# Attention and two dense layers: the product of the last 64 keys in two column halves, and q's rounding and remainder sooner where short units begin

## The reference

```python
scores = scale * np.matmul(q, k.transpose(0, 1, 3, 2))
...
scores = scores + bias.transpose(2, 0, 1)[None, :, :, :]
scores = scores - np.max(scores, axis=-1, keepdims=True)
attn = np.exp(scores)
attn = attn / (np.sum(attn, axis=-1, keepdims=True) + 1e-09)
x = np.matmul(attn, v)            # then the heads side by side: 2304 x 512
h = x @ w_in;  x = (h - np.tanh(h)) @ w_out             # 512 -> 2048 -> 512
g = x @ w_gate
out = (g * (1.0 / (1.0 + np.exp(-g))) * (x @ w_val)) @ w_out2   # 512 -> 1536 -> 512
```

## Time and profile before

| | us |
|---|---|
| median of 3 runs | 1214.85 |
| lowest, highest | 1213.22, 1215.16 |
| the profiled execution | 1216.6 |
| its span, first to last instruction | 1214.7 |
| PE busy | 1179.5 |
| DVE busy | 613.9 |
| ACT busy | 569.4 |
| POOL busy | 527.7 |

### The profile page before, as it was taken

One profiled execution on the slowest core, in us unless ns is written; L12 is line 12 of the kernel. 1 busy time (PEld: TensorE's weight loads), 2 busy tenths in 40 slices (PEclk: granted clock), 3 DMA queues, 4 the chain that ended last, 5 costly groups with the idle time before them and its releaser, 6 DMA issues.

```text
span 1214.7 us, 20186 instructions
## 1 busy us (share of the span) xinstructions
PE 1179.5 (97%) x7320; PEld 1080.2 (89%) x7320; DVE 613.9 (51%) x1377; ACT 569.4 (47%) x1163; POOL 527.7 (43%) x584
## 2 busy tenths in 40 slices
PE   6789999999999999999999999999999999999998
PEld 2356799999999998999999999999999999999998
DVE  8967888766666666666666444321212212121111
ACT  7977676665565556555655544321212112121212
POOL 1057577756565657778777522111111111111111
PEclk9999999999999999999999999999999999999999
DMA  6889565353444335545555433100000000000000
GB/s 199 259 255 266 162 183 152 109 140 109 128 131 125 108 89 159 133 134 138 153 137 139 138 131 130 53 27 27 27 1 27 26 26 26 1 26 1 26 1 26
DMA packets 77763, 125.46 MB, mean 103 GB/s; under 512 B 17120, under 2 KB 40672, under 8 KB 77664
## 3 DMA queue, kind: packets, MB, share of 16 engines
q1 hardware_dynamic: 77664, 124.16, 35.1%
HBM read 104.07 MB, written 20.05 MB: 102 GB/s over the span
## 4 chain that ended last, share of the span: by engine, by line
PE 89%; DVE 5%; ACT 2%; POOL 2%; issue 2%; DMA 0%; DVEq 0%; POOLq 0%; ACTq 0%
PE ps_y L1556 16%; PE ps_h L1537 15%; PE ps_s L1672 12%; PE ps_y L1683 12%; PE ps_s L1454 6%; PE ps_h L1672 6%; PE ps_pt L1672 6%; PE ps_pt L1508 5%; PE ps_pt L1473 5%; DVE feat L1139 3%; PE ps_pt L1537 1%; PE ps_pt L1483 1%; ACT feat L807 1%; PE ps_y L1495 1%; DVE prob L1174 1%
## 5 line engine op out<-in xcount | busy, mean ns | idle before, releaser
L772 POOL TENSOR_TENSOR fr<-tanh_b,fr 128x384 fp32r<-128x384 f32 x72 | 73.2, 1016 | 377.9 <-ACT fr L1066 377.9
L1556 PE MATMUL ps_y<-fr,wbuf 128*128 128x384 f32 x1152 | 230.0, 337 | 0.0
L1537 PE MATMUL ps_h<-fr,wbuf 128*128 128x384 f32 x1056 | 206.3, 338 | 0.3 <-DVE fr L1224 0.3
L1556 PEld LDWEIGHTS ps_y<-fr,wbuf 128*128 128x128 f32 x1152 | 198.2, 188 | 0.7 <-POOL fr L709 0.7
L1537 PEld LDWEIGHTS ps_h<-fr,wbuf 128*128 128x128 f32 x1056 | 181.7, 188 | 1.3 <-issue 0.8
L837 ACT ACTIVATE prob<-prob,negmax 128x576 f32<-128x576 f32 (+1 forms) x160 | 124.0, 775 | 122.9 <-DVE negmax L1174 122.2
L704 POOL TENSOR_SCALAR prob<-prob,rowinv 128x576 f32<-128x576 f32 (+1 forms) x160 | 134.0, 839 | 89.1 <-DVE rowinv L1185 88.9
L1683 PE MATMUL ps_y<-wbuf,fr 128*128 128x512 f32 x648 | 161.1, 393 | 0.0
L709 POOL TENSOR_TENSOR fr<-g_b,fr 128x384 fp32r<-128x384 f32 x96 | 100.6, 1047 | 139.2 <-ACT fr L868 139.2
L1683 PEld LDWEIGHTS ps_y<-wbuf,fr 128*128 128x128 f32 x648 | 120.5, 188 | 22.1 <-POOL fr L772 0.2
L1190 DVE TENSOR_TENSOR wbuf<-ps_pt,wbuf 128x512 fp32r<-128x512 f32 (+1 forms) x136 | 91.6, 673 | 52.4 <-ACT wbuf L851 48.0
(11 more groups left out here) (134 smaller groups left out, 1948.7 us busy)
## 6 DMA issues: line engine op xcount, KB each, us to landing
biasb<-bias_scratch SPq DMA_DIRECT2D x64, 288.0 KB, 3.2
raw<-k_t SPq DMA_DIRECT2D x59, 288.0 KB, 3.0
biasb<-bias_scratch SPq DMA_DIRECT2D x64, 216.0 KB, 2.9
bias_scratch<-w_raw SPq DMA_DIRECT2D x72, 144.0 KB, 3.4
biasb<-bias_scratch SPq DMA_DIRECT2D x64, 144.0 KB, 3.0
w_raw<-w_chunks SPq DMA_DIRECT2D x16, 512.0 KB, 5.1
prob<-w_chunks SPq DMA_DIRECT2D x8, 768.0 KB, 4.3
raw<-v_p SPq DMA_DIRECT2D x36, 160.0 KB, 2.3
```

What stands on the lines that cost most here:

```text
L1537: mm = eng.matmul(hidden_bank(u, c)[:, 0:TOK], w[:, cols], x[:, d, :], start=d == 0 and i == 0, stop=d == KC - 1 and i == 2)
L1556: mm = eng.matmul(ps_y[:, d, 0:TOK], w[:, cols], g[c % 2], start=c == 0 and i == 0, stop=c == C1 - 1 and i == 2)
```

## The change

In the first slot of a unit with 16 heads (`short` with `first`), ScalarE's `q_high` moves from behind `exp_tile(q, 0)` to in front of `pt_high(v, 1)`, and VectorE's `q_low` from behind `score(q, 1)` to in front of `pt_low(v, 1)`. In `output_plain`, the matmul of the last 64 keys, one of 384 tokens into partitions 0 to 63, becomes two of 192 tokens: the first half of the tokens into partitions 0 to 63, the second half into partitions 64 to 127. The stop flag goes from L1495's last matmul to these two.

```diff
@@ scalar, short() @@
                 if first:
                     y_out(u - 1, [0])
+                    q_high(p, moe)
                     pt_high(v, 1, moe)
                     exp_tile(q, 0)
-                    q_high(p, moe)
                     y_out(u - 1, [1, 2, 3])
@@ vector, short() @@
                 if first:
                     score(q, 0, moe)
+                    q_low(p, moe)
                     pt_low(v, 1, moe)
                     inverse(q, 0)
                     score(q, 1, moe)
-                    q_low(p, moe)
                     x_out(v, moe)
@@ tensor, output_plain() @@
                         eng.matmul(bank[64 * i:64 * i + 64, :], v[:, c + i, :], plain_of(hd)[:, c + i, :],
-                                   start=c == 0, stop=i == 1 and c == FULL - 2)
+                                   start=c == 0, stop=False)
                 eng.wait_ge(v_pt, splits(hd, 0) + 1)
-                mm = eng.matmul(bank[0:64, :], v[64:P, FULL, :], plain_end(hd), start=False, stop=True)
+                for i in range(2):
+                    half = slice(i * TOK // 2, (i + 1) * TOK // 2)
+                    mm = eng.matmul(bank[64 * i:64 * i + 64, half], v[64:P, FULL, :], plain_end(hd)[:, half],
+                                    start=False, stop=True)
                 mm.then_inc(e_o, 1)
```

## The result

| | before | after |
|---|---|---|
| median of 10 executions each, us | 1213.46 | 1212.09 |
| lowest, highest | 1213.22, 1215.82 | 1211.04, 1214.66 |
| ratio after / before | | 0.9984, interval 0.9976 to 0.9992 |
| profiled execution, its span | 1216.6, 1214.7 | 1212.36, 1210.5 |

The changed kernel is 1.4 us (0.11%) faster by the medians and 1.9 by the ratio. The forecast, 1213.2, is 1.1 us above the median. The two profiled executions differ by 4.24 us, three times as much, so most of this part asks which share of that is the change.

What follows compares the result with a forecast made beforehand. PE, with 89% of the chain, was taken to bound the kernel. From the three-run median 1214.85 us, -1.04 for the split product and -0.60 for the earlier q gave 1213.2 us, range 1211.0 to 1215.0.

Steps and rivals of the forecast that it cites:

- part 1: Stage without layers: the last 64 keys' product in two column halves, forecast at -1.04 us.
- Part 2: Units where short ones begin: q_high and q_low sooner, forecast at -0.60 us, 0.40 in one unit and 0.20 in the other.
- The size of a product: Last 64 keys' matmul: overlapping column halves take 0.32 us off each product; bounds -0.36 to +0.1.
- Rival C: Last 64 keys' product: the 64-row halves don't overlap and their split gives 0, 1214.25 us; chance 0.08.
- How many count: Stage without layers: five products on the chain, 1.60 us, less 0.32 at head 6 and 0.24 for bias rows: 1.04.
- Head 6 (B): Head 6: q_low comes first, its collision with POOL's L681 goes, 1.1 us more reach the end, 1212.1; chance 0.25.
- A: The forecast itself, 1213.2 us, with q_low (L1146) stretched again at head 6; chance 0.42.
- Bias rows (D): Heads 4 to 7: bias rows come last, not PE; only the first product's 0.32 us gets through, 1213.9; chance 0.12.
- E: Units where short ones begin: the path through tanh and L709 isn't late next, each gives 1.03 us, 1211.7; chance 0.08.
- What is late next: First short unit: second tile's transposes wait for the normalising, which comes 0.40 us earlier, so 1.03 us shrink to 0.40.
- Slower (F): Waits of PE for POOL: 1.14 us becomes some 1.5, half-clock stretches cost 1.7 us each; two plus a collision, 1217.8; chance 0.05.
- The start of the sum: Median of three runs of the kernel before, 1214.85 us, from which the forecast effects were subtracted.

Runs made afterwards that it cites:

- e_low_only: Kernel before with only VectorE's q_low moved before pt_low(v, 1), q_high where it was: median 1216.71 us against 1213.50, ratio 1.0019.
- e_low_after_pt: Changed kernel with q_low one place later, behind pt_low(v, 1), in the first slot of units 4 and 5: median 1211.16 us, ratio to the kernel before 0.9980.
- e_norm_first: Changed kernel with POOL doing norm(q, 1) before split_g in the first slot of units 4 and 5: median 1211.97 us, ratio to the kernel before 0.9987.
- e_product: Kernel before with only the last 64 keys' matmul split into two column halves: median 1211.51 us against 1213.93, ratio 0.9983.
- e_before_again: Kernel before, unchanged, run again: median 1213.89 us against 1213.93, ratio 1.0002.
- e_high_only: Kernel before with only ScalarE's q_high moved before pt_high(v, 1), q_low where it was: median 1214.43 us against 1213.50, ratio 0.9999.
- e_q: Kernel before with only the moves of q_high and q_low, last 64 keys' product as before: median 1212.67 us against 1213.93, ratio 0.9998.
- e_one_half: Changed kernel with both 192-token matmuls in the same column half, so without overlap: median 1212.64 us, ratio to the kernel before 0.9995.
- e_low_early: Changed kernel with VectorE's q_low before score(q, 1) in the heads without layers: median 1212.30 us, ratio to the kernel before 0.9985.
- e_after_again: Changed kernel, unchanged, run again beside the kernel before: median 1212.34 us against 1213.61, ratio 0.9990.
- e_forced: Kernel before with a wait holding VectorE's q_low at head 6 until POOL's k_high is done: median 1213.75 us against 1213.50, ratio 1.0003.

## Why the traces say 4.24 us and the executions 2.1

The second product of the edge slot is one point that each trace has. Its start in PE's timeline of e_low_only (no part 1):

```profile
119.61 1.51 PE L1495 MATMUL ps_y<-w_raw 128*64 128x384 f32 x8 [0.50 <-DVE xy_stage L1215]
```

and of e_low_after_pt (part 1), both executions without a late start, a drop of the clock or a late q_low at heads 6 and 7:

```profile
118.19 1.51 PE L1495 MATMUL ps_y<-w_raw 128*64 128x384 f32 x8 [0.50 <-DVE xy_stage L1215]
```

1.42 us, and 0.31 for the product that starts there: part 1 is worth 1.73 us in the stage. By e_norm_first (118.07) it would be 1.85; the quiet executions of e_product say 1.78. Before it is at 122.85, after at 119.36. The difference of 3.49, and 0.31 again, makes 3.80. Three events lie in it or beside it:

- **A late start, 0.9 to 1.0 us**, in the profiled executions of before, after, e_product, e_before_again and e_high_only and not in the nine others. In before the matmuls of L1439 between 12.4 and 16.2 us last 687 ns at the median, in e_low_only 406. A group of sixteen in PE's timeline of before:

```profile
13.79 2.18 PE L1439 MATMUL ps_y<-feat,prob 128*32 128x288 f32 x16
```

  and in that of e_low_only:

```profile
13.38 1.21 PE L1439 MATMUL ps_y<-feat,prob 128*32 128x288 f32 x16 [0.26 <-issue]
```

  That looks like the lower clock lasting some 4 us longer; the granted clock in the view of that stretch reads 1.00 in both, so this cause is argued and not shown. For it speaks that each trace's list of grants begins, at the full clock, at 15.6 to 16.4 us in these five and at 10.2 to 12.3 in the nine others; what was granted before isn't in the list. Before and after both have it, and it cancels.
- **The clock at half for 3.42 us near 77 us**, in before, e_before_again, e_high_only, e_q, e_one_half and e_low_early: with part 1 and without, always ahead of the first changed product. Score tile (2, 2) starts 0.46 us later in e_low_only than in e_low_after_pt, and 2.89 later in before, of which 1.00 is the late start: 1.43 us for the drop. e_one_half against e_low_only gives 1.32 at this tile, and the executions above 1.4.
- **Late bias rows with the q_low behind them**, 0.8 us at head 6 in before (122.85 - 119.61 = 3.24, less 1.00 and 1.43; against e_high_only, which has the late start and the drop too and the same code here, 1.1: 122.85 - 121.76), 0.87 at head 7 in e_after_again.

So 3.80 = 1.73 (part 1) + 1.43 (drop) + 0.81 (bias rows and collision) - 0.17, which the trace after lost to smaller waits for bias rows and a slightly later start. The prices of the three events are good to some 0.2 us. Part 2 adds 0.40 and 0.16, less 0.12 of shifts between 126 us and the end: 4.24. Only 1.73 + 0.56 = 2.3 of it is the change; the quiet executions show 2.1.

By the medians the gain is 1.3 to 1.4 us, less than by the quiet ones, because fewer executions of the changed kernel were quiet (4 of 10 and 3 of 11; before 6 of 10, and 15, 20 and 20 of 33), while e_low_after_pt, whose stage without layers is the same, had 8 of 11. The event at head 7 is one way to the upper level. Whether part 1 makes it more frequent stays open: some score of heads 1 to 7 waits over 0.1 us for bias rows in six of the seven traces with part 1 and in three of the seven without its overlap, and that is too few to tell.

## Why the prediction was right, and where not

- **The size of a product**: 0.32 us less, right, by e_one_half the overlap alone. Rival C is out.
- **How many count**: 1.04 us was too little; 1.73 measured in the stage, 1.78 in e_product. The step that failed is the deduction of 0.56 us (0.32 behind head 6, 0.24 for the bias rows of head 5). The five products on the chain give 1.60, and a clean execution loses none of them; another 0.13 to 0.25 is unexplained. I had deducted for waits of the one profiled execution, which few others share.
- **Head 6 (B)**: q_low came first after, as B described, but e_q shows the same without part 1. B's mechanism was right and its cause, the shift by part 1, not needed. Its 1.1 us more stands in the profiled pair as 0.8 to 1.1 and not in the quiet executions. By the sign that the prediction names for B (L1146 at 0.5 to 0.9 us) the trace after is B; A and B can't be told apart by that one trace.
- **Bias rows (D)**: they come late in nine of the fourteen traces, at one to three heads, and not in heads 4 to 7 in all. The first product isn't the only one that gets through.
- **Part 2**: 0.60 forecast, 0.56 in the traces, 0.52 in executions. 0.40 in unit 4 to the hundredth; 0.16 for 0.20 in unit 5, with q_low at 0.91 us. E is out.
- **What is late next** was sized rightly and named in part. The transposes of the second tile do wait for the normalising, as forecast, and start 0.06 us after it; the hidden layer ahead of them waits for gated too, which the prediction didn't name. e_norm_first removed the first of these waits for no gain. Both hang on gated, and gated came 0.40 us earlier.
- **The stretched q_low of the earlier trace rows**: the prediction says that it behaves as a lock of whoever starts first. By the row q_low started 0.02 us before L681 and still lost, so that row alone doesn't show it; e_forced and the earlier trace rows do.
- **Slower (F)**: half of 3.42 us, 1.7, was too much for a stretch at half clock, which costs 1.3 to 1.4. PE's wait before the last transposes went from 1.14 to 1.17 us, not to 1.5, with no clock lost (PE's timeline after):

```profile
113.60 0.65 PE L1473 MATMUL ps_pt<-ident,prob 128*128 128x128 f32 x4 [1.17 <-POOL prob L704]
```

- **The start of the sum**: 1214.85, the median of three, was two executions of an upper level and one quiet one. Ten gave 1213.46, 1.4 us less. This is the term behind the miss of 1.1: from 1213.46 the forecast effect of 1.64 gives 1211.8, and the median is 1212.09. That 1.64 lies near the medians' 1.37 is in part luck: part 1 was put 0.7 us too low, and the medians show 0.75 less than the quiet executions of the same comparison, for another reason, the levels.

## What to carry to other kernels

Where a kernel's own executions differ by 3 us, an effect of 2 us isn't read from two profiled executions: pair executions without events, and find each event's price from two traces of the same code. A deduction for a wait belongs in the sum only if the wait is there in most executions, and one profile can't say so. When a small instruction of VectorE lies near one of GpSimd, look at which starts first: a few hundredths of a microsecond decided who was stretched, and moving it by one place was worth 0.2 us here.

## What was not expected of the hardware

- Two matmuls of 192 columns on the same 64 rows and in different column halves run at the same time: four records in 0.47 us, against 0.79 in one half.
- Two engines, one pair of instructions: q_low of 0.56 us and POOL's L681 of 1.41 become 1.76 and 1.41, or 0.56 and 1.79, by a difference in start of 0.06 or 0.05 us. The loser ends its own length less some 0.14 us after the winner, and up to 0.03 us ahead by the record q_low still lost.
- The same instructions had the clock at half for 3.42 us near 77 us in some executions and not in others, at a price of 1.3 to 1.4 us.
